# Where the table pieces are halved: one, one, one, three and nine in five bodies instead of three in each

## The chip, the cores and the metric

The kernel runs on one core of a Trainium2 chip. The metric is the device time of one execution in microseconds (us), lower is better; several runs give a median. Engines: PE is TensorE, DVE is VectorE, ACT is ScalarE, POOL is GpSimd, SP is SyncE, which only issues DMAs here.

## The reference

An attention with a recurrent state per head, then two channel stages on its output. B=4, H=8, S=768, D=40:

```
state = 0                                   # per batch and head, D x D
for t in range(S):
    y[t]  = r[t] @ state
    Sa    = state @ a[t]
    state = state * w[t] - outer(Sa, b[t]) + outer(v[t], k[t])
x = y as (B, S, 320)
h = relu(x @ w_in)                          # 320 -> 1024
x = (h * sigmoid(conv3(h))) @ w_out         # 1024 -> 320
u = x + real(fft(fft(x, axis=1), axis=2))
x = u + relu(norm(u) @ w_ch1) @ w_ch2       # 320 -> 1280 -> 320
```

## The kernel before

**Two parts.** `attention` (line 141) runs for the first half of the time, `channels` (line 832) for the rest. The channel stages multiply each operand as a high and a low part (a rounded value and what is left of it), so their weights and Fourier tables have to be split too. That splitting is done during the attention: the tables lie in DRAM side by side (`in_tables`), cut into 17 pieces (`PIECES`, lines 38 and 39): pieces 0 to 12 of 998 columns, piece 13 of 358, pieces 14 to 16 (the last tiles) of 768, all on 128 partitions.

**A piece** takes three jobs. `fetch` (line 344, SP): load it into `w_in`. `halve` (line 433, POOL): `high` = rounded copy (a CAST, L436), then the piece minus `high` in place (L438). `put` (line 352, SP): store `high` (L356) and, after the subtraction, the low part (L358) into the scratch tensors `high_scratch` and `low_scratch`; the last tiles go to `last_scratch` (L360, L362). The place is the buffer of `w` (`w_in`): `piece(i)` (line 263) gives its first and second n columns. It is free between the scans of one step's `w` and the load of the next `w`. `fetch` waits until all scans so far are done (`s_decay`) and until all earlier puts have landed (`s_put`, 32 per piece); `load_w` (line 284) waits for the puts too.

**The attention in bodies.** Time is cut into 6 steps of 128 tokens, each of two chunks of 64. `attention_jobs` (line 80) makes one list of jobs from four words lists: `START`, then `STEP` once for each of g = 0 to 4 (the five *bodies*), then `LAST`. The list is written out by hand and says for every engine in which order it works: each engine walks through the whole list and does its own share, so a job that waits holds all later jobs of its engine. The first number of a word is the step relative to g: `sat:0` belongs to step g, `ta:1` to the preparation of step g+1, `scan:2` to step g+2. Words for steps past the last are dropped, so the fifth body has no scan, `at`, `keys`, `gram`, `decays` and no loads for them. PSUM has six rotating banks, taken in list order.

What stands near the change, by step and chunk:

- `xn` (xi): TensorE multiplies `z` and `kb_tok` (L806), VectorE adds the state (L571), then POOL multiplies it by `w_end` (L445) and counts `s_x`. Four quarters per chunk.
- `xt` (L826, TensorE, transposes of xi) waits for two of the chunk's four POOL products (line 823), the second for four. `sat` (L784, TensorE) of the next chunk: its first half needs two, its second half four (line 780).
- `sub`: VectorE's elimination, 31 pairs of L544 and L546 per step; `unsplit` its two transposes (L553, L558). `diag`: POOL (L456) and ACT (L621) copy `inv_d` into `inv_t`. `mj` (L752), `mt` (L761) and `pu` (L772) follow on TensorE; `pu` needs both copies. `sat` of the next step follows `pu`.
- `keys` (L432, POOL): `kb` times `after`, and `at` (L422, POOL): `a` times `decay`, both before `gram` (L735, TensorE).
- `st` (L799), `y` (L819, L821; VectorE L578) and, on SP, the stores of y for the second chunk (L380). `chunk`: SP loads `rt` and `zt` of the next chunk (L279, L280), once `y` of this chunk is in PSUM.
- `tables` in `LAST` (line 383): SP loads y back and, after all puts, the first weights from the scratch tensors.

In the fifth body the pieces 14, 15 and 16 stand as fetch:0, fetch:1 and fetch:2 do in every body: on POOL `halve:0` behind the four `xn` of the first chunk, `halve:1` ahead of the last three `xn` of the second, `halve:2` behind `diag`. In the numbering of the jobs:

```
number = n[0] + 2 + 3 * g if g >= 0 else n[0]
if number < len(PIECES):
    out.append((stage, 0, 0, number))
```

Of the kernel before, what the change touches and what calls it, by code (L numbers as in the profile page):

```python
# [8 lines left out]
F32 = mybir.dt.float32  # L9
F32R = mybir.dt.float32r  # L10
FP8 = mybir.dt.float8e4

NB, NH, S, D = 4, 8, 768, 40
# [4 lines left out]
STEPS = S // (2 * C)  # L18
# [19 lines left out]
PIECES = [("whole", lo, min(lo + 998, WHOLE)) for lo in range(0, WHOLE, 998)]  # L38
PIECES += [("last", lo, lo + 768) for lo in range(0, LAST_TILES, 768)]

# [26 lines left out]
sub:2 decays:2:0:2 pu:1:1:3 sub:2 pu:1:1:2 xt:0:1:1 sub:2 pu:1:0:3 sub:2 sub:2 sub:2 sub:2 sub:2 pu:1:0:2 sub:2 sub:2  # L70
sub:2 pu:1:1:1 weights:3:0:0 chunk:1:1:0 sub:2 sub:2 sub:2 sub:2
"""
LAST = """
sat:0:0:0 sat:0:0:1 sa:0:0:1 st:0:0:0 sa:0:0:0 xn:0:0:1 xn:0:0:0 sa:0:0:2 st:0:0:1 y:0:0:0 tables:0:0:0 sat:0:1:0
sa:0:0:3 y:0:0:1 st:0:1:0 xt:0:0:0 xn:0:0:2 xn:0:0:3 y:0:1:0 st:0:0:3 st:0:0:2 y:0:0:3 y:0:0:2 rows:0:0:0 sat:0:1:1
# [4 lines left out]
def attention_jobs():  # L80
    solved = [0] * STEPS

    def jobs(words, g):
        out = []
        for word in words.split():
            stage, *numbers = word.split(":")
            n = [int(x) for x in numbers]
            step = g + n[0]
            if stage in ("fetch", "halve", "put"):
                number = n[0] + 2 + 3 * g if g >= 0 else n[0]  # L90
                if number < len(PIECES):
                    out.append((stage, 0, 0, number))
            elif step >= STEPS:
                continue
            elif stage == "sub":
                out.append((stage, step, 0, solved[step]))
                solved[step] += 1
            else:
                job = (stage, step, n[1], n[2])
                out.append(("part", job, n[3], 2) if len(n) > 3 else job)  # L100
        return out

    order = jobs(START, -1)
    for g in range(STEPS - 1):
        order += jobs(STEP, g)
    order += jobs(LAST, STEPS - 1)


    families = {}
    for job in order:  # L110
        if job[0] in UNITS or job[0] in COUNTED:
            families.setdefault(job[:2] if job[0] == "pu" else job[:3], []).append(job)
    numbered = {}
    for family in families.values():
        numbered.update(zip(family, sorted(family, key=lambda job: (job[3], job[2]))))
    return [("part", numbered[job[1]], *job[2:]) if job[0] == "part" else numbered.get(job, job) for job in order]
# [24 lines left out]
def attention(nc, ctx, dram, tables, kept):  # L141
# [4 lines left out]
    def sem(name):  # L146
        return ctx.enter_context(nc.semaphore(name))
# [58 lines left out]
    s_at = sem("s_at")  # L206
# [13 lines left out]
    s_chain = sem("s_chain")  # L220
    s_x = sem("s_x")

    s_fetch = sem("s_fetch")
    s_phigh = sem("s_phigh")
    s_plow = sem("s_plow")
    s_put = sem("s_put")
    s_xin = [sem(f"s_xin{i}") for i in range(2)]
    s_x0hi = sem("s_x0hi")

# [33 lines left out]
    def piece(i):  # L263
        table, lo, hi = PIECES[i]
        n = hi - lo
        return table, lo, hi, w_in[:, 0:n], w_in[:, n:2 * n].bitcast(F32R)

    block = ctx.enter_context(nc.Block())

# [1 line left out]
    def _(sp):  # L271
# [12 lines left out]
        def load_w(g):  # L284
            if g:

                sp.wait_ge(s_decay, NB * g)
            if g > 1:
                fill_of(sp, ("pu", g - 2, 1, NB - 1))
            if halved[0]:  # L290
                sp.wait_ge(s_put, 32 * halved[0])
            for b in range(NB):
                cols = slice(b * NH * SEG + (b > 0), (b + 1) * NH * SEG + 1)
                sp.dma_start(w_in[:, cols], dram["w"][g, :, cols]).then_inc(s_w[b], 16)
# [42 lines left out]
        for stage, g, c, b in whole:  # L337
# [6 lines left out]
            if stage == "fetch":  # L344

                sp.wait_ge(s_decay, NB * scanned)
                if b:
                    sp.wait_ge(s_put, 32 * b)
                table, lo, hi, x, high = piece(b)
                sp.dma_start(x, dram["tables"][:, lo + (WHOLE if table == "last" else 0):hi + (WHOLE if table == "last" else 0)]  # L350
                             ).then_inc(s_fetch, 16)
            if stage == "put":
                table, lo, hi, x, high = piece(b)
                sp.wait_ge(s_phigh, b + 1)
                if table == "whole":
                    sp.dma_start(dram["high"][:, lo:hi], high.bitcast(F32)).then_inc(s_put, 16)  # L356
                    sp.wait_ge(s_plow, b + 1)
                    sp.dma_start(dram["low"][:, lo:hi], x).then_inc(s_put, 16)  # L358
                else:
                    sp.dma_start(dram["last"][0:64, lo:hi], high[0:64].bitcast(F32)).then_inc(s_put, 16)  # L360
                    sp.wait_ge(s_plow, b + 1)
                    sp.dma_start(dram["last"][64:128, lo:hi], x[64:128]).then_inc(s_put, 16)  # L362
                halved[0] += 1
            if stage == "scan":
                scanned = g + 1
# [17 lines left out]
            if stage == "tables":  # L383

                fill_of(sp, ("pu", STEPS - 1, 1, NB - 1))
                sp.wait_ge(s_at, 2 * STEPS)
                sp.wait_ge(s_bt, NB * STEPS)
                sp.wait_ge(s_wp, NB * STEPS)
                sp.wait_ge(s_end, 2 * STEPS)
                load_rows(0)  # L390
                sp.wait_ge(s_put, 32 * len(PIECES))
                for k, part in enumerate(("high", "low")):
                    sp.dma_start(w1[:, k, 0:2, :].rearrange("p t f -> p (t f)").bitcast(F32), dram[part][:, 0:W1]).then_inc(s_w1, 16)
                sp.dma_start(w1[:, 0, 2, :].bitcast(F32), dram["last"][:, 0:FF]).then_inc(s_w1, 16)
# [8 lines left out]
    def _(pool):  # L403
# [9 lines left out]
        for job in whole:  # L413
# [18 lines left out]
                    nc.gpsimd.tensor_tensor(x, x, by, ALU.mult).then_inc(done, 1)  # L432
            elif stage == "halve":
                table, lo, hi, x, high = piece(b)
                pool.wait_ge(s_fetch, 16 * (b + 1))
                nc.gpsimd.tensor_copy(high, x).then_inc(s_phigh, 1)  # L436
                pool.wait_ge(s_phigh, b + 1)
                nc.gpsimd.tensor_tensor(x.bitcast(F32R), x, high.bitcast(F32), ALU.subtract).then_inc(s_plow, 1)  # L438
            elif stage == "xn":

                drain_of(pool, job)
                pool.wait_ge(s_end, 2 * (g + c) + 2)
                state = xi[0:D, b * NH:(b + 1) * NH, 0:D]
                ends = w_end[:, (g + c) % 2, b * NH:(b + 1) * NH, 1 - c]
                nc.gpsimd.tensor_tensor(state, state, ends.unsqueeze(2).broadcast_to([D, NH, D]),  # L445
                                        ALU.mult).then_inc(s_x, 1)
            elif stage == "diag":

                pool.wait_ge(s_zero, 2)
                pool.wait_ge(s_inv, g + 1)  # L450
                if g:

                    fill_of(pool, ("pu", g - 1, 1, NB - 1))
                for cc in range(2):
                    p = C * cc
                    nc.gpsimd.tensor_copy(inv_t_pairs[p:p + Q, :, :, cc, 0:Q], inv_d_slots(p, cc)).then_inc(s_diag_low, 1)  # L456
                    pool.wait_ge(s_diag_low, 2 * g + cc + 1)
# [1235 lines left out]
```

## Time and profile before

| | us |
|---|---|
| median of 3 runs (932.67 to 942.92) | 937.42 |
| the profiled execution | 942.25 |
| its span, first to last instruction | 940.5 |
| busy: PE, DVE, ACT, POOL | 859.7, 610.7, 412.8, 179.5 |
| attention, up to the start of the channel part | about 464.4 |

A row of a timeline gives the start, the time from the first start to the last end, engine, line, operation, tiles written and read, and how many instructions were merged; in brackets how long the engine idled before and what ended that. PEclk is the granted TensorE clock as a share of 2.4 GHz. A landing time of a DMA counts from its issue. A DMA's own duration on SP is how long the issue held the queue. Body 1 runs from about 94.5 to 165.5 us, body 2 to 234.5, body 3 to 306, body 4 to 376.5 and body 5 to 434.5.

### The profile page before, as it was taken

What the parts mean: (1) busy time and instruction counts of PE and PEld (TensorE: products, weight loads), DVE (VectorE), ACT (ScalarE), POOL (GpSimd) and SP (SyncE); (2) the same over time, 40 slices, a digit from 0 to 9 for tenths busy, and PEclk for the clock granted to TensorE, in tenths of its full rate; (3) what the DMA queues carried; (4) which work ended last, traced back from release to release, by engine and by line L of the source; (5) the groups of instructions that cost most, each with busy time, mean ns of one, the idle gap of its engine ahead of it and who ended that gap; (6) DMA issues with size and microseconds to landing.
All of it is one profiled execution on the core that took longest, in us unless ns stands there. A gap on an engine that the chain in (4) does not pass through costs nothing.

```text
span 940.5 us, 26345 instructions
## 1 busy us (share of the span) xinstructions
PE 859.7 (91%) x11113; PEld 819.8 (87%) x11113; DVE 610.7 (65%) x1215; ACT 412.8 (44%) x784; POOL 179.5 (19%) x195
## 2 busy tenths in 40 slices
PE   0769989989989989989899899999999999999998
PEld 0669878888889889979888799999999999999998
DVE  8895877877877876551476746757367574775522
ACT  1565337337346346334266245632455234652311
POOL 5260381381371380240000000000000000000000
PEclk9878999999997997978999999999999999999999
DMA  9751473574564572254880010000100020000000
GB/s 314 218 184 47 144 248 135 187 249 166 175 233 150 186 236 89 49 160 139 299 342 1 1 52 22 1 1 27 47 22 1 1 72 1 22 2 1 22 22 22
DMA packets 58677, 100.79 MB, mean 107 GB/s; under 512 B 28529, under 2 KB 40562, under 8 KB 54898
## 3 DMA queue, kind: packets, MB, share of 16 engines
q1 hardware_dynamic: 58562, 99.11, 32.0%
q8 instruction: 90, 1.47, 0.7%
q14 instruction: 25, 0.20, 0.1%
HBM read 76.40 MB, written 22.70 MB: 105 GB/s over the span
## 4 chain that ended last, share of the span: by engine, by line
PE 40%; DVE 8%; ACT 1%; issue 1%; DVEq 0%; ACTq 0%
PE psum L1393 19%; PE psum L1453 9%; PE psum L1419 8%; PE psum L1473 2%; DVE stats L1262 1%; PE psum L1489 1%; DVE res L1272 1%; DVE hid L1208 1%; DVE res L1253 1%; DVE tok L1264 1%; DVE xn L1197 1%; DVE cv L1285 1%; DVE res L1254 1%; DVE cv L1283 1%; DVE gs L1203 0%
## 5 line engine op out<-in xcount | busy, mean ns | idle before, releaser
L1393 PE MATMUL psum<-xn,w 128*128 128x384 f32 x640 | 125.1, 339 | 0.2 <-DVE xn L1197 0.2
L1393 PEld LDWEIGHTS psum<-xn,w 128*128 128x128 f32 x640 | 110.5, 188 | 1.1 <-issue 0.6
L1393 PE MATMUL psum<-xs,w 128*128 128x384 f32 x512 | 97.3, 343 | 5.9 <-PEq L1604 3.7
L1393 PEld LDWEIGHTS psum<-xs,w 128*128 128x128 f32 x512 | 91.5, 194 | 6.3 <-issue 6.3
L1419 PE MATMUL psum<-w,gs 128*128 128x320 f32 x576 | 90.0, 310 | 4.2 <-DVE gs L1203 4.1
L1419 PEld LDWEIGHTS psum<-w,gs 128*128 128x128 f32 x576 | 86.3, 188 | 5.9 <-DVE gs L1203 5.9
L735 PE MATMUL bank<-at,kb 64*64 64x64 f32 x1536 | 51.8, 238 | 36.7 <-DVE kb L506 21.3
L735 PEld LDWEIGHTS bank<-at,kb 64*64 64x64 f32 x1536 | 47.0, 148 | 40.4 <-issue 33.3
L445 POOL TENSOR_TENSOR xi<-xi,w_end 40x320 f32<-40x320 f32 x44 | 31.0, 723 | 208.1 <-DVE xi L571 177.1
L546 DVE TENSOR_TENSOR inv<-inv,outer 128x31 f32<-128x31 f32 (+15 forms) x186 | 64.9, 349 | 6.4
L563 DVE TENSOR_TENSOR score<-bank,mask 128x512 f32<-128x512 f32 x48 | 32.7, 690 | 55.2 <-PE bank L799 54.5
L1283 DVE SCALAR_TENSOR_TENSOR cv<-hp,conv,cv 128x768 f32<-128x768 f32 x32 | 32.6, 1018 | 52.4 <-ACT cv L1094 52.4
L544 DVE TENSOR_TENSOR outer<-low,inv 128x31 f32<-128x31 f32 (+15 forms) x186 | 62.4, 335 | 5.0
L772 PE MATMUL bank<-inv_t,rhs 128*80 128x128 f32 x384 | 60.0, 327 | 3.1 <-issue 3.1
L1453 PE MATMUL psum<-w,hid 128*128 128x320 f32 x360 | 59.9, 311 | 2.3 <-DVE res L1272 1.3
L1453 PE MATMUL psum<-w,gs 128*128 128x320 f32 x360 | 60.0, 311 | 0.0
L772 PEld LDWEIGHTS bank<-inv_t,rhs 128*80 128x80 f32 x384 | 55.9, 188 | 4.4 <-issue 3.8
L1453 PEld LDWEIGHTS psum<-w,hid 128*128 128x128 f32 x360 | 54.9, 188 | 4.6 <-DVE hid L1208 2.8
L432 POOL TENSOR_TENSOR kb<-kb,after 128x512 f32<-128x512 f32 x44 | 53.5, 1243 | 20.0 <-DMA kb<-in_kb 19.9
L1453 PEld LDWEIGHTS psum<-w,gs 128*128 128x128 f32 x360 | 55.4, 188 | 1.2 <-DVE gs L1208 1.0
L1208 DVE SCALAR_TENSOR_TENSOR gs<-psum,gs 128x384 fp32r<-128x384 f32 x40 | 22.3, 557 | 52.0 <-ACT gs L1073 52.0
L799 PE MATMUL bank<-rt,zt 128*128 128x128 f32 x384 | 53.7, 284 | 0.5 <-DVE y_t L578 0.5
(129 smaller groups left out, 1674.9 us busy)
## 6 DMA issues: line engine op xcount, KB each, us to landing
kb<-in_kb SPq DMA_DIRECT2D x24, 512.0 KB, 8.2
rt<-in_rt SPq DMA_DIRECT2D x12, 1024.0 KB, 8.5
w_in<-in_tables SPq DMA_DIRECT2D x13, 499.0 KB, 3.6
high_scratch<-w_in SPq DMA_DIRECT2D x13, 499.0 KB, 3.3
low_scratch<-w_in SPq DMA_DIRECT2D x13, 499.0 KB, 3.8
at<-in_a SPq DMA_DIRECT2D x6, 1024.0 KB, 4.9
zt<-in_vt SPq DMA_DIRECT2D x12, 512.0 KB, 9.6
w_in<-in_w SPq DMA_DIRECT2D x18, 260.0 KB, 4.5
```

The source lines that it names most:

```text
L432: nc.gpsimd.tensor_tensor(x, x, by, ALU.mult).then_inc(done, 1)
L544: link(nc.vector.tensor_tensor(prod, low[:, b + 1:Q, b:b + 1].broadcast_to([128, n, m]), inv[:, b:b + 1, 0:m].broadcast_to([128, n, m]), A ...
L546: link(nc.vector.tensor_tensor(inv[:, b + 1:Q, 0:m], inv[:, b + 1:Q, 0:m], prod, ALU.add))
L563: nc.vector.tensor_tensor(score[:, b * NH:(b + 1) * NH, :], bank, mask[:, :].unsqueeze(1).broadcast_to([128, NH, C]), ALU.mult).then_inc(d ...
L735: last = mm(out[C * cc:C * cc + C, i, :], kb[r, n, cc, c, :], at_chunks[r, n, cc, :], start=True, stop=True)
L772: last = mm(t[0:2 * D, 128 * i:128 * i + 128], rhs[:, h, :], inv_t[:, h, :, :], start=True, stop=True)
L799: last = mm(t[:, 128 * i:128 * i + 128], zt[:, c, n, :], rt[:, c, n, :, :], start=True, stop=True)
L1208: nc.vector.scalar_tensor_tensor(hid[q % 2][:, f % 2, 1, :], ps[6 + f % 2][:, 0:HALF], 0.0, f32(hid[q % 2][:, f % 2, 0, :]), ALU.max, ALU. ...
L1283: link(nc.vector.scalar_tensor_tensor(cv[:, :], h[:, 1:S + 1], conv[:, f, 1:2], cv[:, :], ALU.mult, ALU.add))
L1393: last = mm(ps[bank][:, 0:HALF], a[:, 128 * f:128 * f + 128], y[:, HALF * half:HALF * (half + 1)], start=(i == 0), stop=(i == len(every) - 1))
L1419: last = mm(ps[t][:, 0:DM], gs[:, f % 2, x, 128 * t:128 * t + 128], w2[:, y, f, :], start=(f == 0 and m == 0), stop=(f == NF - 1 and m == 2))
L1453: last = mm(ps[HALVES[k]][:, 0:DM], hid[h][:, f % 2, x, 128 * k:128 * k + 128], w4[:, y, f, :], start=(f == 0 and m == 0), stop=(f == NC - ...
```

## The change

The pieces keep their order and their jobs. The start still does two. Bodies 1, 2 and 3 do one each, at the place of their old fetch:0, halve:0 and put:0. Body 4 does three, in the old places. Body 5 does nine (pieces 8 to 16) and has its own list, `LATE`, in which the other jobs stand in the same order as in `STEP`. Since no `w` and no `decay` is needed any more then, the nine take turns in two places, `w_in` and `decay`, with a semaphore each for fetch and put. A fetch waits for the earlier puts of its own place only; one into `decay` also waits for all `decays` copies (`s_wp`) and all `at` products (`s_at`).

```diff
--- before.py
+++ after.py
@@ -37,6 +37,10 @@
 WHOLE, LAST_TILES = W1 + W2 + DFT_S + DFT_D + W3 + W4, FF + FC
 PIECES = [("whole", lo, min(lo + 998, WHOLE)) for lo in range(0, WHOLE, 998)]
 PIECES += [("last", lo, lo + 768) for lo in range(0, LAST_TILES, 768)]
+
+BY_STEP = (2, 1, 1, 1, 3, 9)
+TURNS = sum(BY_STEP[:-1])
+assert len(PIECES) == sum(BY_STEP)
 
 
 
@@ -70,6 +74,19 @@
 sub:2 decays:2:0:2 pu:1:1:3 sub:2 pu:1:1:2 xt:0:1:1 sub:2 pu:1:0:3 sub:2 sub:2 sub:2 sub:2 sub:2 pu:1:0:2 sub:2 sub:2
 sub:2 pu:1:1:1 weights:3:0:0 chunk:1:1:0 sub:2 sub:2 sub:2 sub:2
 """
+LATE = """
+fetch:0 fetch:1 sat:0:0:0 ta:1:0:0 halve:0 put:0 sat:0:0:1 sa:0:0:1 ta:1:0:1 tb:1:1:3 sa:0:0:0 ta:1:0:3 ta:1:0:2
+st:0:0:0:0 st:0:0:0 fetch:2 halve:1 put:1 akv:1:0:0:0 akv:1:0:0 st:0:0:1:0 st:0:0:1 sa:0:0:3 tb:1:1:2 akv:1:0:1:0
+akv:1:0:1 st:0:0:2:0 xn:0:0:0 fetch:3 halve:2 put:2 st:0:0:2 st:0:0:3:0 akv:1:0:2:0 akv:1:0:2 st:0:0:3 akv:1:0:3:0
+sub:1 sa:0:0:2 tb:1:1:1 tb:1:1:0 fetch:4 halve:3 put:3 akv:1:0:3 xn:0:0:2 xn:0:0:1 xn:0:0:3 y:0:0:0:0 y:0:0:0
+y:0:0:1:0 y:0:0:1 sub:1 tb:1:0:0 fetch:5 halve:4 put:4 tb:1:0:1 y:0:0:2:0 y:0:0:2 xt:0:0:1 tb:1:0:3 sub:1 sat:0:1:1
+sub:1 sub:1 sub:1 fetch:6 halve:5 put:5 sub:1 sat:0:1:0 sub:1 y:0:0:3:0 y:0:0:3 chunk:1:0:0 xt:0:0:0 sa:0:1:0 sa:0:1:1
+fetch:7 halve:6 put:6 sa:0:1:3 st:0:1:1:0 xn:0:1:0 st:0:1:1 sub:1 tb:1:0:2 sa:0:1:2 st:0:1:0:0 st:0:1:3:0 sub:1
+fetch:8 halve:7 put:7 st:0:1:0 st:0:1:2:0 st:0:1:2 st:0:1:3 sub:1 xn:0:1:1 sub:1 xn:0:1:2 xn:0:1:3 y:0:1:0:0 halve:8
+put:8 y:0:1:1:0 y:0:1:2:0 y:0:1:1 y:0:1:0 sub:1 sub:1 sub:1 unsplit:1:0:0 y:0:1:2 y:0:1:3:0 y:0:1:3 diag:1:0:0
+mj:1:0:0:0 mj:1:0:1:0 mj:1:0:1 mj:1:0:0 mt:1:0:0:0 mt:1:0:0 xt:0:1:0 pu:1:0:0 pu:1:1:0 mt:1:0:1:0 mt:1:0:1 pu:1:0:1
+pu:1:1:3 pu:1:1:2 xt:0:1:1 pu:1:0:3 pu:1:0:2 pu:1:1:1 chunk:1:1:0
+"""
 LAST = """
 sat:0:0:0 sat:0:0:1 sa:0:0:1 st:0:0:0 sa:0:0:0 xn:0:0:1 xn:0:0:0 sa:0:0:2 st:0:0:1 y:0:0:0 tables:0:0:0 sat:0:1:0
 sa:0:0:3 y:0:0:1 st:0:1:0 xt:0:0:0 xn:0:0:2 xn:0:0:3 y:0:1:0 st:0:0:3 st:0:0:2 y:0:0:3 y:0:0:2 rows:0:0:0 sat:0:1:1
@@ -87,9 +104,8 @@
             n = [int(x) for x in numbers]
             step = g + n[0]
             if stage in ("fetch", "halve", "put"):
-                number = n[0] + 2 + 3 * g if g >= 0 else n[0]
-                if number < len(PIECES):
-                    out.append((stage, 0, 0, number))
+                if n[0] < BY_STEP[g + 1]:
+                    out.append((stage, 0, 0, sum(BY_STEP[:g + 1]) + n[0]))
             elif step >= STEPS:
                 continue
             elif stage == "sub":
@@ -101,8 +117,9 @@
         return out
 
     order = jobs(START, -1)
-    for g in range(STEPS - 1):
+    for g in range(STEPS - 2):
         order += jobs(STEP, g)
+    order += jobs(LATE, STEPS - 2)
     order += jobs(LAST, STEPS - 1)
 
 
@@ -220,10 +237,10 @@
     s_chain = sem("s_chain")
     s_x = sem("s_x")
 
-    s_fetch = sem("s_fetch")
+    s_fetch = [sem(f"s_fetch{i}") for i in range(2)]
     s_phigh = sem("s_phigh")
     s_plow = sem("s_plow")
-    s_put = sem("s_put")
+    s_put = [sem(f"s_put{i}") for i in range(2)]
     s_xin = [sem(f"s_xin{i}") for i in range(2)]
     s_x0hi = sem("s_x0hi")
 
@@ -263,7 +280,15 @@
     def piece(i):
         table, lo, hi = PIECES[i]
         n = hi - lo
-        return table, lo, hi, w_in[:, 0:n], w_in[:, n:2 * n].bitcast(F32R)
+        where = decay if turn(i) else w_in
+        return table, lo, hi, where[:, 0:n], where[:, n:2 * n].bitcast(F32R)
+
+    def turn(i):
+        return (i - TURNS) % 2 if i >= TURNS else 0
+
+    def fellows(i):
+
+        return sum(turn(k) == turn(i) for k in range(i + 1))
 
     block = ctx.enter_context(nc.Block())
 
@@ -288,7 +313,7 @@
             if g > 1:
                 fill_of(sp, ("pu", g - 2, 1, NB - 1))
             if halved[0]:
-                sp.wait_ge(s_put, 32 * halved[0])
+                sp.wait_ge(s_put[0], 32 * halved[0])
             for b in range(NB):
                 cols = slice(b * NH * SEG + (b > 0), (b + 1) * NH * SEG + 1)
                 sp.dma_start(w_in[:, cols], dram["w"][g, :, cols]).then_inc(s_w[b], 16)
@@ -344,22 +369,25 @@
             if stage == "fetch":
 
                 sp.wait_ge(s_decay, NB * scanned)
-                if b:
-                    sp.wait_ge(s_put, 32 * b)
+                if turn(b):
+                    sp.wait_ge(s_wp, NB * STEPS)
+                    sp.wait_ge(s_at, 2 * STEPS)
+                if fellows(b) > 1:
+                    sp.wait_ge(s_put[turn(b)], 32 * (fellows(b) - 1))
                 table, lo, hi, x, high = piece(b)
                 sp.dma_start(x, dram["tables"][:, lo + (WHOLE if table == "last" else 0):hi + (WHOLE if table == "last" else 0)]
-                             ).then_inc(s_fetch, 16)
+                             ).then_inc(s_fetch[turn(b)], 16)
             if stage == "put":
                 table, lo, hi, x, high = piece(b)
                 sp.wait_ge(s_phigh, b + 1)
                 if table == "whole":
-                    sp.dma_start(dram["high"][:, lo:hi], high.bitcast(F32)).then_inc(s_put, 16)
+                    sp.dma_start(dram["high"][:, lo:hi], high.bitcast(F32)).then_inc(s_put[turn(b)], 16)
                     sp.wait_ge(s_plow, b + 1)
-                    sp.dma_start(dram["low"][:, lo:hi], x).then_inc(s_put, 16)
+                    sp.dma_start(dram["low"][:, lo:hi], x).then_inc(s_put[turn(b)], 16)
                 else:
-                    sp.dma_start(dram["last"][0:64, lo:hi], high[0:64].bitcast(F32)).then_inc(s_put, 16)
+                    sp.dma_start(dram["last"][0:64, lo:hi], high[0:64].bitcast(F32)).then_inc(s_put[turn(b)], 16)
                     sp.wait_ge(s_plow, b + 1)
-                    sp.dma_start(dram["last"][64:128, lo:hi], x[64:128]).then_inc(s_put, 16)
+                    sp.dma_start(dram["last"][64:128, lo:hi], x[64:128]).then_inc(s_put[turn(b)], 16)
                 halved[0] += 1
             if stage == "scan":
                 scanned = g + 1
@@ -388,7 +416,8 @@
                 sp.wait_ge(s_wp, NB * STEPS)
                 sp.wait_ge(s_end, 2 * STEPS)
                 load_rows(0)
-                sp.wait_ge(s_put, 32 * len(PIECES))
+                for k in range(2):
+                    sp.wait_ge(s_put[k], 32 * sum(turn(i) == k for i in range(len(PIECES))))
                 for k, part in enumerate(("high", "low")):
                     sp.dma_start(w1[:, k, 0:2, :].rearrange("p t f -> p (t f)").bitcast(F32), dram[part][:, 0:W1]).then_inc(s_w1, 16)
                 sp.dma_start(w1[:, 0, 2, :].bitcast(F32), dram["last"][:, 0:FF]).then_inc(s_w1, 16)
@@ -432,7 +461,7 @@
                     nc.gpsimd.tensor_tensor(x, x, by, ALU.mult).then_inc(done, 1)
             elif stage == "halve":
                 table, lo, hi, x, high = piece(b)
-                pool.wait_ge(s_fetch, 16 * (b + 1))
+                pool.wait_ge(s_fetch[turn(b)], 16 * fellows(b))
                 nc.gpsimd.tensor_copy(high, x).then_inc(s_phigh, 1)
                 pool.wait_ge(s_phigh, b + 1)
                 nc.gpsimd.tensor_tensor(x.bitcast(F32R), x, high.bitcast(F32), ALU.subtract).then_inc(s_plow, 1)
```

## Rows read from the trace of the kernel before

**Rows 1.** Busy time by stretch; columns: stretch, length, busy of each engine (instructions), PEclk, DMA share, GB/s.
```profile
94.50:165.50 71.00, 63.80 (x1394) 58.95 (x1390) 55.12 (x114) 33.69 (x69) 29.88 (x26) 0.98 0.53 179
165.50:234.50 69.00, 64.39 (x1411) 59.33 (x1407) 54.92 (x114) 33.57 (x69) 29.87 (x26) 0.98 0.60 197
234.50:306.00 71.50, 67.45 (x1390) 62.49 (x1388) 54.66 (x113) 33.93 (x69) 29.90 (x26) 0.90 0.57 188
...
376.50:434.50 58.00, 53.42 (x1036) 50.29 (x1035) 25.55 (x56) 20.91 (x41) 15.52 (x16) 0.85 0.33 84
```

**Rows 2.** Timeline of POOL, second body: the first halving, the last keys.
```profile
183.42 1.02 POOL L436 CAST w_in<-w_in 128x998 fp32r<-128x998 f32 x1 [0.73 <-DMA w_in<-in_tables]
184.51 1.96 POOL L438 TENSOR_TENSOR w_in<-w_in 128x998 fp32r<-128x998 f32 x1
...
200.29 2.34 POOL L432 TENSOR_TENSOR kb<-kb,after 128x512 f32<-128x512 f32 x2 [2.01 <-DMA kb<-in_kb]
```

**Rows 3.** Timeline of SP, second body: the last `kb` load and the next fetch.
```profile
191.39 5.33 SPq L312 DMA_DIRECT2D kb<-in_kb  x1
196.82 1.35 SPq L350 DMA_DIRECT2D w_in<-in_tables  x1
```

**Rows 4.** Timeline of POOL, fifth body: the xi products and the diagonal copy.
```profile
383.05 0.72 POOL L445 TENSOR_TENSOR xi<-xi,w_end 40x320 f32<-40x320 f32 x1 [28.49 <-DVE xi L571]
389.29 2.10 POOL L445 TENSOR_TENSOR xi<-xi,w_end 40x320 f32<-40x320 f32 x3 [5.51 <-DVE xi L571]
...
415.24 2.12 POOL L456 COPY inv_t<-inv_d 32x1024 f32<-32x1024 f32 x2 [4.06 <-issue]
```

**Rows 5.** Timeline of PE, fifth body: xt, sat, mj and the first pu.
```profile
393.61 0.69 PE L826 MATMUL bank<-ident,xi 40*128 40x40 f32 x8
...
394.82 2.08 PE L784 MATMUL bank<-pu,xi 80*64 80x64 f32 x64
...
413.52 3.47 PE L752 MATMUL bank<-inner,gram_m 32*32 32x32 f32 x128 [2.63 <-DVE inner L553]
...
421.86 3.67 PE L772 MATMUL bank<-inv_t,rhs 128*80 128x128 f32 x16 [0.30 <-issue]
```

**Rows 6.** Timeline of SP, fifth body: two fetches, rt ahead of the second, rt after the last pu.
```profile
371.76 3.65 SPq L350 DMA_DIRECT2D w_in<-in_tables  x1
...
397.84 0.34 SPq L279 DMA_DIRECT2D rt<-in_rt  x1
...
398.91 3.81 SPq L350 DMA_DIRECT2D w_in<-in_tables  x1
...
435.35 0.36 SPq L279 DMA_DIRECT2D rt<-in_rt  x1
```

**Rows 7.** Single DMAs and their landing times, issued near 144, 286, 372 and 399.
```profile
low_scratch<-w_in SPq DMA_DIRECT2D x1, 499.0 KB, 5.2
...
low_scratch<-w_in SPq DMA_DIRECT2D x1, 499.0 KB, 2.6
...
w_in<-in_tables SPq DMA_DIRECT2D x1, 384.0 KB, 7.1
...
w_in<-in_tables SPq DMA_DIRECT2D x1, 384.0 KB, 7.4
```

**Rows 8.** The page's DMA issues: median time to landing over 13 pieces.
```profile
w_in<-in_tables SPq DMA_DIRECT2D x13, 499.0 KB, 3.6
...
low_scratch<-w_in SPq DMA_DIRECT2D x13, 499.0 KB, 3.8
```

**Rows 9.** Timeline of DVE: one shape of sub, in the second and the fifth body.
```profile
184.92 0.40 DVE L544 TENSOR_TENSOR outer<-low,inv 128x231 f32<-128x231 f32 x1
...
395.91 0.40 DVE L544 TENSOR_TENSOR outer<-low,inv 128x231 f32<-128x231 f32 x1
```

**Rows 10.** Two stretches of PE alone: stretch, length, busy, PEclk, DMA share, GB/s.
```profile
281.00:295.00 14.00, 13.46 (x200) 0.52 0.38 134
...
414.00:431.00 17.00, 15.05 (x282) 0.50 0.24 65
```

## The prediction

> **What bounds the kernel now.** I read the busy time by stretch first, one stretch per body. TensorE is busy for 63.8 of 71.0 us in the first body, 64.4 of 69.0 in the second and 67.45 of 71.5 in the third: it idles 7.2, 4.6 and 4.0 us. In the fifth it is busy 53.4 of 58.0 us, beside 25.6 us of VectorE and only 15.5 us of GpSimd [rows 1]. So TensorE's own list of jobs sets the time, and another engine counts only where its result comes after TensorE wants it. That is why the rest is read in order of time: for each job on GpSimd and on the queue of SyncE, when it ends and when TensorE asks for it. The profiled execution took 942.25 us (span 940.5, 1.75 around it), the median is 937.42; a shift read in the span is added to the median. A measurement of this kernel can tell about 1% (9.4 us) from no change.
>
> **The first three bodies: two pieces fewer in each.** What stays is the piece at fetch:0, whose halving stands ahead of GpSimd's work on `at` and `kb`. What goes is halve:1 and halve:2. One halving is a cast of 1.02 and a subtraction of 1.96 us, 3.0 together [rows 2], so six of them are 18 us of GpSimd, with three times 0.5 MB of DMA each. Is any of it waited for? The one thing of that part of a body that TensorE needs is the last quarter of `kb`, for which GpSimd waits 2.01 us in the second body [rows 2]. But that load is issued at 191.39 and holds the queue for 5.33 us, and the second piece's fetch goes out behind it, at 196.82 [rows 3]; the pieces that go are all behind the wait, and the one in front of it stays. The halvings that go stand in front of three xi products and the low diagonal copy, or behind it; in the fifth body, with its halvings in the same places, that copy still has 4.5 us of slack [rows 4, 5]. I take 0 for the three bodies. Bounds: a loss has no mechanism there, so 0 at the most above; the gain is bounded by TensorE's 15.8 us of idle time in them [rows 1], far from 0, and this belongs to a rival below. The fourth body keeps three pieces in the old places: 0.
>
> **The fifth body: nine instead of three.** The list without fetch, halve and put is word for word the old one, so only the nine pieces and what waits behind them on SyncE and GpSimd change. Two xi events of the old run matter, because both stand on GpSimd behind halvings now.
>
> First event. GpSimd did the first xi product at 383.05 and the other three from 389.29, 2.10 us in all [rows 4]. TensorE's first xt of this body (two products needed) began at 393.61, the second half of sat (all four) at about 395.9 [rows 5]. Slack: 3.6 and 4.5 us. Now halve:0 and halve:1 stand ahead of the first product, halve:2 and halve:3 ahead of the three. Step by step, with the number of the piece in the list:
> - fetch 0 is issued at 371.76, as now, and holds the queue until 375.4 behind rt and zt [rows 6]. It landed after 7.1 us with 384 KB [rows 7]; with 499 KB I take 7.5: 379.3. Halve 0 ends at 382.3. Fetch 1 (the second place, `decay`) needs nothing but decays and `at` of the last step, both long done; halve 1 ends at 385.3, the first product at 386.0. Nobody waits for that one.
> - put 0 (low half) goes at 382.3 and takes 3.8 [rows 8]: 386.1. Only then may fetch 2 go, 3.6 us [rows 8]: 389.7. Halve 2 ends 392.7.
> - put 1 is issued by SyncE only behind fetch 2. Its low half leaves about 0.8 after that fetch, behind 1 MB of the queue. Bounds: 2.6 alone, 7.1 behind rt and zt; I take 5.2, a low half measured with traffic near it [rows 7]. So put 1 lands 6.0 after fetch 2's issue: 392.1. Fetch 3: 395.7. Halve 3 ends 398.7.
> - The second product of the body ends at 399.4, the fourth at 400.8. TensorE's xt starts 399.4 instead of 393.6: **5.8 us of waiting**. Sat's second half would then stand at 401.7, and is covered.
> VectorE doesn't take this back: after the shift it waits for TensorE's results in the old order, and TensorE still waits 2.63 us for its transpose before mj [rows 5].
>
> Second event. The low diagonal copy ran 415.24 to 417.4 on GpSimd [rows 4], pu wanted it at 421.86 [rows 5]: slack 4.5. Going on with 6.0 per fetch and put, and a second place in between:
> - put 2 398.1, fetch 4 401.7, halve 4 404.7; put 3 404.1, fetch 5 (358 columns, estimated 2.9) 407.0, halve 5 (in proportion 1.3) 408.3; put 4 410.1, fetch 6 (768 columns) 413.7, halve 6 (2.7, estimated between proportion and whole) 416.4.
> - rt and zt for the last step now leave SyncE behind put 5, about 411.4, instead of 397.84; they are wanted in the last body and have time. Fetch 7 stands behind them. Before, the fetch issued 1.07 after rt held the queue 3.81 us [rows 6] and landed after 7.4 [rows 7], 8.5 after rt. So fetch 7 lands 419.9, halve 7 ends 422.6, three xi products 424.7.
> - put 6 leaves when that issue is through, 418.6, and lands 422.4; fetch 8 426.0; halve 8 428.7; diagonal copy (2.12) 430.8.
> TensorE, 5.8 late, would start pu at 427.7; it starts at 430.8: **another 3.1 us**. Together the last body starts 8.9 us late. The y stores wait on SyncE behind put 8 and go from about 429 on; the rows and tables they feed are loaded only once the last pu is filled (435.35 before [rows 6], some 444 now), so they stay covered, and so does the wait for all puts.
>
> Ends of the unknown terms: with every put at the 2.6 to 3.8 of the quiet rows [rows 7, 8] the same walk gives 3.2 for the first wait and 0.8 for the second, 4.0 in all. With 7.1 instead of 5.2 for each of the four crowded puts it gives 8.9 + 4 x 1.9 = 16.5. **Sum: 937.4 + 0 + 5.8 + 3.1 = 946.3 us.**
>
> A rule to weigh. While GpSimd ran the subtraction of a halving (184.51 to 186.47) [rows 2], VectorE's product of 128x231 took 0.40 us; the same shape at 395.91, with GpSimd idle, took 0.40 [rows 9]. The Trainium skill (SBUF — State Buffer, "Who interferes with whom") says that a VectorE instruction with both inputs in SBUF and a GpSimd instruction that reads SBUF shut each other out for a whole instruction. This trace doesn't agree: no stretching at all, so the sum has no such term.
>
> **The rivals.**
> - The puts are quick: only the xi wait is left, 4.0 us, 941.4. For it: 2.6 us landings exist. Against: here put and fetch queue behind one another every time.
> - TensorE's clock. Idle of a few us is followed by half speed here: 281 to 295 at 0.52, 414 to 431 at 0.50 [rows 10]. A wait of 5.8 at 393.6 may bring a stretch like the first, 14 us at 0.52, 6.7 us of work lost, before pu. Then pu starts at 421.9 + 5.8 + 6.7 = 434.4, the second wait is covered, +12.5: 949.9. Against: in the forecast up to 3.1 us of that is hidden behind the GpSimd chain, and VectorE limits part of this stretch anyway.
> - The other side, faster: the fetch behind the last `kb` quarter does share the engines with it. Without it `kb` lands earlier by up to the 2.01 us of GpSimd's wait in each of three bodies [rows 2], 6.0; and where TensorE then idles less, the third body's low-clock stretch [rows 10] goes, 6.7 more. 12.7 against 8.9 is -3.8: 933.6. It decides only if both come. Against it: the order of the queue [rows 3].
> - The pieces move and all stays covered: 937.4. This needs halve 3 to end before 393, three landings faster than any row here.
> - GpSimd and VectorE shut each other out. VectorE limits TensorE only in front of the transpose, where halve 4 and 5 run, 4.3 us: 8.9 + 4.3, 950.6. Rows 9 speak against it.
>
> **How the numbers follow.** Forecast 0.45, quick puts 0.17, clock 0.18, faster bodies 0.10, all covered 0.07, shut out 0.03. The forecast lies 0.95% above before, so about half of it counts as slower by over 1% (0.22); with the clock and the shut-out that is 0.40. Faster by over 1% needs the kb rival and a little more: 0.05. Within 1%: 0.55. The forecast's own range is 941.4 to 953.9; the stated one goes down to 936, which leaves out most of the faster case, and up to 954.
>
> **What would show it.** In the changed profile, the first xt of the fifth body comes 3 to 6 us later against sat of that body, with TensorE idle in front, released by GpSimd's xi product; GpSimd waits for the fetches of pieces 2 and 3 in between. The low diagonal copy ends after TensorE has finished mt, and pu waits for it. Bodies one to three stay at 71, 69 and 71.5 us within 1.5 us each, apart from the clock. I am wrong if the xi products come before TensorE wants them, or if those three bodies shrink by more than 2 us each with GpSimd's wait for `kb` gone.

## The result and the profile after

The changed kernel took 945.64 us (median of 12 executions, 936.9 to 953.32), before 936.11 us (12 executions beside it). The ratio is 1.0072, 95% interval 1.0045 to 1.0098. Some executions of a kernel are slow ones (two of the twelve here), and a ratio leaves them out; by the two medians alone it would be 1.010. Measured a second time beside other kernels it gave 1.0089 (1.0054 to 1.0124). So the changed kernel is slower by 0.7 to 0.9%, 7 to 8 us; the medians differ by 9.5 and 10.3 us.

The profiled execution after took 945.71 us with a span of 943.9; the one before had 940.5. The first view to look at is the busy time by stretch, with the stretches cut as in [rows 1], 6 to 7 us behind the `sat` that opens each body (start and end, length, busy of PE, PEld, DVE, ACT, POOL, then PEclk, DMA share, GB/s):

```profile
94.50:162.50 68.00, 63.83 (x1396) 58.81 (x1394) 55.17 (x114) 33.51 (x69) 24.05 (x22) 0.97 0.43 142
162.50:230.50 68.00, 63.64 (x1402) 58.95 (x1400) 54.78 (x114) 33.62 (x69) 24.00 (x22) 0.97 0.48 156
230.50:298.70 68.20, 63.78 (x1396) 58.83 (x1392) 54.60 (x114) 33.61 (x69) 24.00 (x22) 0.97 0.48 150
298.70:369.40 70.70, 65.41 (x1374) 60.62 (x1371) 51.50 (x110) 33.90 (x69) 29.88 (x26) 0.93 0.57 185
369.40:438.00 68.60, 56.41 (x1037) 52.77 (x1036) 25.59 (x56) 20.93 (x41) 31.37 (x28) 0.80 0.61 190
```

Against [rows 1], GpSimd has 6 us less in each of the first three bodies and 16 more in the fifth. From sat to sat the bodies take 68.1, 67.9, 68.3, 71.8 and 75.2 us, before 71.1, 68.6, 71.8, 71.7 and 64.7. The first three are 7.2 us shorter together, the fifth 10.5 longer; behind it both kernels need the same 505.3 us. Of the 7.2 us, 2.9 are idle time of TensorE (15.9 before, 12.9 after) and 4.3 are busy time, at 0.95 of the clock before and 0.97 after. Two executions of one kernel differ by as much as that gain, as shown further down, so the profile alone proves only the loss.

The timeline of GpSimd in the fifth body shows the chain:

```profile
378.06 0.72 POOL L474 TENSOR_TENSOR xi<-xi,w_end 40x320 f32<-40x320 f32 x1
382.09 1.01 POOL L465 CAST w_in<-w_in 128x998 fp32r<-128x998 f32 x1 [3.31 <-DMA w_in<-in_tables]
383.19 1.95 POOL L467 TENSOR_TENSOR w_in<-w_in 128x998 fp32r<-128x998 f32 x1
390.10 1.01 POOL L465 CAST decay<-decay 128x998 fp32r<-128x998 f32 x1 [4.96 <-DMA decay<-in_tables]
391.19 1.95 POOL L467 TENSOR_TENSOR decay<-decay 128x998 fp32r<-128x998 f32 x1
393.10 2.09 POOL L474 TENSOR_TENSOR xi<-xi,w_end 40x320 f32<-40x320 f32 x3
...
416.86 0.82 POOL L465 CAST decay<-decay 128x768 fp32r<-128x768 f32 x1 [5.46 <-DMA decay<-in_tables]
417.77 1.81 POOL L467 TENSOR_TENSOR decay<-decay 128x768 fp32r<-128x768 f32 x1
419.54 2.09 POOL L474 TENSOR_TENSOR xi<-xi,w_end 40x320 f32<-40x320 f32 x3
421.58 0.81 POOL L465 CAST w_in<-w_in 128x768 fp32r<-128x768 f32 x1
422.47 1.81 POOL L467 TENSOR_TENSOR w_in<-w_in 128x768 fp32r<-128x768 f32 x1
424.22 2.12 POOL L485 COPY inv_t<-inv_d 32x1024 f32<-32x1024 f32 x2
```

GpSimd stands idle for 4.96 us ahead of the fourth halving, waiting for its DMA, and the three xi products stand behind it. In [rows 4] they ran as soon as VectorE had added the state. TensorE pays for it (timeline of PE, the rows with a wait; xt, mj, mt, pu):

```profile
393.96 1.05 PE L855 MATMUL bank<-ident,xi 40*128 40x40 f32 x8 [6.93 <-POOL xi L474]
...
419.70 3.06 PE L781 MATMUL bank<-inner,gram_m 32*32 32x32 f32 x128 [2.64 <-DVE inner L582]
424.84 1.92 PE L790 MATMUL bank<-inv_d,inner 32*32 32x32 f32 x64 [2.08 <-ACT inner L697]
...
428.06 3.28 PE L801 MATMUL bank<-inv_t,rhs 128*80 128x128 f32 x16 [0.30 <-issue]
```

The wait ahead of xt is 6.93 us (none in [rows 5]). The wait ahead of pu isn't there: the diagonal copy ends at 426.34, TensorE arrives at 428.06. It arrives late because its clock fell during the first wait and stayed low behind it (stretch, length, busy, PEclk, DMA share, GB/s):

```profile
383.00:394.00 11.00, 3.82 (x94) 0.81 0.56 174
394.00:408.00 14.00, 14.00 (x156) 0.54 0.71 238
```

The clock is at half speed until 406.9. The kernel before has full speed from 366.0 to 413.8 and half speed from there to 430.9 (see [rows 10]); after, that second stretch is shorter, 420.6 to 430.8. So pu starts 13.3 us later within its body than before, and 2.8 us of that are won back behind it. Of the 10.5 us by which the fifth body grew, 6.9 are the wait, 2.9 more busy time of TensorE (63.0 us against 60.1), and 0.7 other waits.

### The profile page after: what moved, and what is told of

Same layout as the page of the kernel before. It is cut to its first block, busy times and chain, and to the rows that moved or that the text cites. A ratio compares the mean times of both kernels' runs of the same rounds, so it can differ in the third digit from the quotient of the medians.

```text
span 943.9 us, 26345 instructions
## 1 busy us (share of the span) xinstructions
PE 857.0 (91%) x11113; PEld 816.8 (87%) x11113; DVE 610.8 (65%) x1215; ACT 412.0 (44%) x784; POOL 179.7 (19%) x195
## 4 chain that ended last, share of the span: by engine, by line
PE 40%; DVE 8%; ACT 1%; issue 1%; DVEq 0%; ACTq 0%
PE psum L1422 19%; PE psum L1482 9%; PE psum L1448 8%; PE psum L1502 2%; DVE stats L1291 1%; PE psum L1518 1%; DVE res L1301 1%; DVE hid L1237 1%; DVE res L1282 1%; DVE tok L1293 1%; DVE xn L1226 1%; DVE cv L1314 1%; DVE res L1283 1%; DVE cv L1312 1%; DVE gs L1232 0%
## 5 line engine op out<-in xcount | busy, mean ns | idle before, releaser
L575 DVE TENSOR_TENSOR inv<-inv,outer 128x31 f32<-128x31 f32 (+15 forms) x186 | 64.9, 349 | 6.4
L801 PE MATMUL bank<-inv_t,rhs 128*80 128x128 f32 x384 | 56.3, 314 | 3.7 <-issue 3.7
L801 PEld LDWEIGHTS bank<-inv_t,rhs 128*80 128x80 f32 x384 | 52.5, 179 | 4.9 <-issue 4.3
```

The lines of the kernel that those rows point to most:

```text
L575: link(nc.vector.tensor_tensor(inv[:, b + 1:Q, 0:m], inv[:, b + 1:Q, 0:m], prod, ALU.add))
L801: last = mm(t[0:2 * D, 128 * i:128 * i + 128], rhs[:, h, :], inv_t[:, h, :, :], start=True, stop=True)
```

## The experiments

All ratios are to the kernel before, run on the same chip in turns.

**1. The loss alone.** Three pieces stay in bodies 1 to 3, and the fifth does the nine of the changed kernel.

```diff
-BY_STEP = (2, 1, 1, 1, 3, 9)
+PIECES = PIECES[0:14] + PIECES[8:17]
+BY_STEP = (2, 3, 3, 3, 3, 9)
```

> Bodies 1 to 4 keep three pieces each as before; the fifth does the nine of the changed kernel (pieces 8 to 16, of which 8 to 13 are done a second time with the same values). Bodies are measured from sat to sat on TensorE: before 71.1, 68.6, 71.8, 71.7, 64.7 us, after 68.1, 67.9, 68.3, 71.8, 75.2. Theory (the gain in bodies 1 to 3 comes from the pieces that are gone): bodies 1 to 3 as before, sum 209 to 214, the fifth 74 to 77, so 9 to 12 us slower than before, and some 7 slower than the changed kernel minus noise of 3. Rival (the shorter bodies are luck of TensorE's clock in one execution): no difference from the changed kernel beyond noise, 5 to 8 us slower than before.

Measured: 1.0139 (1.0099 to 1.0180), six executions. Bodies 72.4, 72.2, 68.8, 68.1, 72.0. The first three sum to 213.4, as expected. The fifth is shorter than the 74 to 77 expected, while the total, 13 us, is just over the 9 to 12 expected.

> loss_only again. First measurement 1.0139 (1.0099 to 1.0180) on six runs. Theory by the steps of the prediction: 8.9 us or 1.0095; what the profiles show beyond it, a crowded put of 7.5 us instead of 5.2 and half speed behind the first wait, allows up to 1.015. In the profile a wait of 5.5 to 7.5 us ahead of the first xt.

Measured: 1.0093 (1.0056 to 1.0129). Bodies 70.2, 68.0, 68.4, 68.4, 74.1. Both are slower than before by 9 to 13 us, and both profiles have both waits, ahead of xt and of pu: 5.91 and 0.99 us in the first, 6.82 and 1.88 in the second:

```profile
391.12 1.04 PE L856 MATMUL bank<-ident,xi 40*128 40x40 f32 x8 [6.82 <-POOL xi L475]
...
423.86 3.67 PE L802 MATMUL bank<-inv_t,rhs 128*80 128x128 f32 x16 [1.88 <-POOL inv_t L486]
```

**2. The gain alone.** One piece in bodies 1 to 3, three in the fourth and fifth, six not done. The diff leaves out the stores of constants that fill the place of the six, and that the fifth body has the old list again.

```diff
-BY_STEP = (2, 1, 1, 1, 3, 9)
+PIECES = [PIECES[i] for i in (0, 1, 2, 5, 8, 11, 12, 13, 14, 15, 16)]
+BY_STEP = (2, 1, 1, 1, 3, 3)
```

> One piece in each of bodies 1 to 3, three in the fourth and fifth as before; the six pieces that have gone are not done at all, their columns of the scratch tensors are filled with constants in the start (12 stores of 0.5 MB), so the output is not the reference's. Theory: bodies 1 to 3 take 68 us each, sum 203 to 206 against 211.5 before, the fifth 64 to 66, total 5 to 8 us faster than before. Rival (clock luck): sum 208 to 214, total within 2 us of before.

Measured: 0.9981 (0.9951 to 1.0011). Bodies 67.1, 71.3, 71.3, 71.2, 62.0. The first three sum to 209.7 and the total is 2 us from before: this measurement alone is what the rival expected.

> gain_only again. First measurement 0.9981 (0.9951 to 1.0011). Theory (less traffic in bodies 1 to 3, fewer stops of TensorE in the middle of a job): 0.994 to 0.999; rival (no gain at all): 0.999 to 1.002.

Measured: 0.9950 (0.9915 to 0.9984). Bodies 70.9, 68.0, 68.3, 71.8, 64.8. The mean of both is 0.9966, 3 us. There is a gain, smaller than the 7.2 us of the one profile, and below the 5 to 8 us first expected.

**3. Which part of a piece costs time in bodies 1 to 3.** Both kernels are built so that the part that stays is at its old place.

```diff
 halves_stay: as gain_only
+                if stage == "halve" and 0 <= g < 3 and n[0] > 0:
+                    out.append(("idle", 0, 0, 2 * g + n[0] - 1))
 ...
+            elif stage == "idle":
+                nc.gpsimd.tensor_copy(high, x).then_inc(s_ihigh, 1)
 ...
+                nc.gpsimd.tensor_tensor(x.bitcast(F32R), x, high.bitcast(F32), ALU.subtract).then_inc(s_ilow, 1)
 traffic_stays: (2, 3, 3, 3, 3, 3), BARE = (3, 4, 6, 7, 9, 10)
 ...
             elif stage == "halve":
+                if b in BARE:
+                    continue
```

> As gain_only, but GpSimd does the six halvings in bodies 1 to 3 at their old places, on what lies in w_in, with no fetch and no put (same computation left out as there). Theory A (the gain comes from the DMA traffic of the pieces, which delays TensorE's instruction fetch and other loads): as gain_only, sum of bodies 1 to 3 203 to 206. Theory B (the gain comes from GpSimd's time, behind which xi products and the diagonal copy stand): as before, 209 to 213, total 0 to 2 us from before.

Measured: 0.9958 (0.9930 to 0.9987). Bodies 67.7, 68.0, 68.2, sum 203.9, as theory A expected.

> Three pieces in every body as before, but for the second and third piece of bodies 1 to 3 GpSimd does nothing: they are fetched and put without being halved, so the low part is the whole value and the high part is stale and the output is not the reference's. Theory A (traffic): as before, sum of bodies 1 to 3 209 to 213, total within 2 us of before. Theory B (GpSimd's time): sum 203 to 206, total 5 to 8 us faster.

Measured: 1.0032 (0.9998 to 1.0066). Bodies 74.9, 75.0, 70.6, sum 220.4. That is well over the 209 to 213 expected: the granted clock of this one execution was 0.89, 0.89 and 0.95 in them, so the sum says little and the time decides. The time is 3 us over before, where at most 2 were expected; its interval reaches down to no change.

The two ratios were measured on one chip and their intervals don't meet. Theory A: the 18 us of GpSimd's work cost nothing, the DMA traffic does. Where, the list of waits of TensorE says (us in total, times, longest). Over 94 to 305 us, before:

```profile
PE bank L735 <- issue: 4.9, 4, 1.9
PE bank L752 <- issue: 2.3, 3, 1.1
```

traffic_stays, the same two jobs (gram and mj):

```profile
PE bank L773 <- issue: 8.9, 6, 2.8
PE bank L790 <- issue: 3.5, 3, 1.8
```

halves_stay (gram is L787, mj L804):

```profile
PE bank L787 <- issue: 1.5, 3, 1.0
...
PE bank L804 <- issue: 1.2, 2, 1.0
```

These are stops in which TensorE waits for no semaphore that the profile shows, and they stand in the middle of a job. Before, first body:

```profile
129.68 0.56 PE L735 MATMUL bank<-at,kb 64*64 64x64 f32 x10
132.02 0.44 PE L735 MATMUL bank<-at,kb 64*64 64x64 f32 x6 [1.78 <-issue]
...
139.55 1.26 PE L752 MATMUL bank<-inner,gram_m 32*32 32x32 f32 x67
141.50 1.14 PE L752 MATMUL bank<-inner,gram_m 32*32 32x32 f32 x61 [0.70 <-issue]
```

After, same place:

```profile
129.76 0.56 PE L764 MATMUL bank<-at,kb 64*64 64x64 f32 x10
131.28 0.44 PE L764 MATMUL bank<-at,kb 64*64 64x64 f32 x6 [0.96 <-issue]
...
137.33 1.26 PE L781 MATMUL bank<-inner,gram_m 32*32 32x32 f32 x67
139.46 1.14 PE L781 MATMUL bank<-inner,gram_m 32*32 32x32 f32 x61 [0.87 <-issue]
```

The job is cut at the same instruction in both kernels (10 and 6, 67 and 61), whatever the length of the stop. All stops without a releaser in bodies 1 to 3 add up to 11.7, 13.9, 8.9 and 14.1 us in the four profiles with three pieces (before, loss_only twice, traffic_stays), and to 4.6 to 6.0 us in the nine with one (5.4 and 6.0 in the changed kernel, 5.9, 5.5 and 5.3 in gain_only twice and halves_stay). In each sum 1.3 to 2.1 us stand ahead of the first pu of a body, whatever the traffic.

What ends the others can be read from the traces. The page of the kernel before lists, beside the queue that moves the data, a DMA queue of another kind, with packets of 16 KB:

```profile
q1 hardware_dynamic: 58562, 99.11, 32.0%
q8 instruction: 90, 1.47, 0.7%
```

In bodies 1 to 3 such a packet comes about every 6 us. Over all thirteen profiles the timeline of TensorE from 86 to 450 us shows 141 stops without a releaser other than those ahead of pu, of 0.15 to 2.83 us, and every one of them ends 1.19 to 1.65 us after the end of a packet of this queue. The stop of 1.78 us above ends at 132.02, its packet ran from 129.78 to 130.71. The stop of 0.96 us ends at 131.28, its packet ran from 128.97 to 129.90. The packet took 0.93 us both times, it only began 0.8 us later. So TensorE stands there for want of its next instructions. Why the packet begins later where the traffic is heavier, no run here shows.

Not all of this is paid. From three pieces to one the stops shrink by 6.7 us in the mean of the profiles, but all idle time of TensorE in bodies 1 to 3 only from 15.6 to 13.3 us (means of four and nine profiles): where TensorE stops less, it waits longer for others, in the changed profile 2.3 us instead of 0.8 for ScalarE's copy of `gram_m`. That is the size of the 3 us in the times.

**4. Is it one wait or a chain?** The fourth halving alone moved behind the three xi products.

```diff
-... tb:1:1:0 fetch:4 halve:3 put:3 akv:1:0:3 xn:0:0:2 xn:0:0:1 xn:0:0:3 ...
+... tb:1:1:0 fetch:4 put:3 akv:1:0:3 xn:0:0:2 xn:0:0:1 xn:0:0:3 halve:3 ...
```

> The changed kernel, with only the halving of the fifth body's fourth piece (halve:3) moved from ahead of that body's last three xi products of the first chunk to behind them. Theory (two gates on one self-timed chain of fetch, halve and put): the wait of 6.9 us ahead of xt goes, but the low diagonal copy stays behind halve:8, which ends near 424 whatever TensorE does, so pu waits instead; the fifth body 72 to 75 us against 75.2 after, 0 to 3 us faster than the changed kernel. Rival (only the first wait mattered, the slack of 4.5 us of the diagonal copy holds): fifth body 65 to 67 us, 8 to 10 us faster than the changed kernel.

Measured: 1.0075 (1.0046 to 1.0103), the changed kernel's time. Its profile is of an execution with a span of 953.7, far above its median, so only who waits for whom is read from it:

```profile
396.86 0.66 PE L855 MATMUL bank<-ident,xi 40*128 40x40 f32 x8 [0.49 <-POOL xi L474]
...
429.53 1.05 PE L855 MATMUL bank<-ident,xi 40*128 40x40 f32 x8 [4.96 <-POOL xi L474]
435.72 3.67 PE L801 MATMUL bank<-inv_t,rhs 128*80 128x128 f32 x16 [5.15 <-POOL inv_t L485]
```

The first wait is 0.49 us instead of 6.93, no low clock follows it (1.00 from 390 to 410 us), and its time comes back at the next two places where TensorE meets a product that stands behind a halving. The chain of fetch, halve and put runs at its own pace; removing one gate moves the wait to the next.

**5. All gates.** halve:2 and halve:3 behind the xi products, halve:6, 7 and 8 behind the diagonal copy; fetches and puts untouched. The cut shows where they stand now; each is still done once.

```diff
-... xn:0:0:3 ...
+... xn:0:0:3 halve:2 halve:3 ...
-... diag:1:0:0 ...
+... diag:1:0:0 halve:6 halve:7 halve:8 ...
```

> The changed kernel, with halve:2 and halve:3 behind the xi products of the first chunk and halve:6, halve:7 and halve:8 behind the low diagonal copy in GpSimd's order; fetches and puts keep their order on SyncE. Theory: no halving that waits for a DMA stands ahead of a product that TensorE wants; the fifth body takes 64 to 67 us, both waits gone, all puts landed by about 425, ahead of the load of the tables; 8 to 11 us faster than the changed kernel, and 1 to 4 us faster than before. Rival (the traffic of six more pieces itself stops TensorE in the fifth body, as it did in bodies 1 to 3): fifth body 68 to 72 us.

Measured: 0.9989 (0.9960 to 1.0018). Bodies 67.9, 71.5, 68.2, 75.2, 63.6.

> all_moved again, beside late_place on the same chip. Fifth body 63 to 66 us with no wait on GpSimd's products; total within 3 us of before.

Measured: 1.0010 (0.9976 to 1.0045). Bodies 68.1, 67.7, 68.2, 68.3, 64.3. The fifth body is as short as before with the nine pieces in it, GpSimd's products are no longer waited for, and the rival (68 to 72 us) is out. The kernel is 6 to 9 us faster than the changed one by the ratios, and not to be told from the one before.

The gain of 1 to 4 us over before, as expected, did not come, although gain_only and halves_stay (0.9981, 0.9950, 0.9958) have it with the same one piece in bodies 1 to 3. Part of the cost went along with the pieces: the stops without a releaser in the fifth body are 1.0 and 1.7 us here against 0.3 before, and behind that body the kernel needs 506.1 us in both profiles, against 505.3. The rest is no larger than the intervals and stays open.

These two profiles are of one and the same kernel, and its fourth body took 75.2 in one and 68.3 in the other. The stretch of that body (length, busy of PE, PEclk, DMA share, GB/s), first all_moved, then all_moved_b:

```profile
294.40:369.60 75.20, 69.44 (x1395) 0.89 0.54 179
```

```profile
291.00:359.40 68.40, 63.98 (x1394) 0.98 0.61 197
```

The clock was granted for 0.89 and for 0.98 of full speed: 69.4 us of busy time against 64.0, for the same matmuls. A body of this kernel that takes 71 or 75 us instead of 68 is no evidence on a change.

**6. The one piece at a quieter place.**

```diff
-                if n[0] < BY_STEP[g + 1]:
+                if 0 <= g < 3:
+                    if n[0] == 2:
+                        out.append((stage, 0, 0, sum(BY_STEP[:g + 1])))
+                elif n[0] < BY_STEP[g + 1]:
```

> As all_moved, and the one piece of bodies 1, 2 and 3 is done at the old place of the third (fetch:2, halve:2 behind the diagonal copy, put:2) instead of the first. Theory (what TensorE loses in these bodies is the DMA traffic of pieces in the stretch of kb loads and short matmuls): GpSimd's waits for kb shrink from 2.0, 1.5 and 2.3 us to under 1 each, bodies 1 to 3 take 66 to 68 us each, total 2 to 5 us faster than all_moved, so 3 to 6 faster than before. Rival: one piece at that place stops TensorE in mj and mt instead, sum of bodies 1 to 3 within 2 us of all_moved, no difference in time.

Measured: 0.9988 (0.9958 to 1.0017), medians 936.61 and 937.63 for all_moved_b beside it. Bodies 70.3, 66.3, 71.3. GpSimd's waits for `kb` are 1.69, 0.92 and 1.92 us, against 2.45, 2.49 and 3.65 in all_moved_b: shorter, and nothing in the time follows from it. TensorE's stops without a releaser in bodies 1 to 3 are 4.7 us, against 4.6 and 5.5 in the two profiles of all_moved, so the new place doesn't spare them. The expected 2 to 5 us were a miss.

**7. Do the parts add up?**

> The changed kernel again, beside loss_only and gain_only on one chip, to see whether the two parts add up. If they do: its ratio to before is that of loss_only plus that of gain_only minus 1, within 0.004. First measurement 1.0072, so 1.004 to 1.010.

Measured: 1.0089 (1.0054 to 1.0124). Means of two measurements each: loss 1.0116, gain 0.9966, sum less one 1.0082; changed kernel 1.0081. Over all measurements they add up: about 11 us lost in the fifth body, 3 won in the first three. The last three, taken on one chip, do so less well: 1.0093 and 0.9950 would give 1.0043, which is 0.0046 from 1.0089 and so just outside the 0.004 expected. Each ratio is known to about 0.0035, so this doesn't contradict the sum, but it doesn't show it either, and it leaves the 3 us uncertain by as much.

## Why the prediction was right, and where not

The forecast was 946.3, measured 945.64; in change, 8.9 us against 6.7 and 8.3 by the two ratios, 9.5 and 10.3 by the medians. Its main mechanism, GpSimd's products held up behind halvings that wait for their DMAs, is the one seen. Point by point:

- **The first event, 5.8 us.** The wait is there, on the product named, and measures 6.93, 5.91, 6.82 and 5.54 us in four profiles with the nine pieces (after, loss_only twice, changed_b). The walk through the chain can be laid beside the changed profile, in which fetch 0 is issued 7.2 us earlier (364.55):

| start of | predicted, less 7.2 | measured |
|---|---|---|
| halve 0 | 372.1 | 372.06 |
| halve 2 | 382.5 | 382.09 |
| halve 3 | 388.5 | 390.10 |
| halve 4 | 394.5 | 396.77 |
| halve 6 | 406.5 | 408.01 |
| halve 7 | 412.7 | 416.86 |
| end of the diagonal copy | 423.6 | 426.34 |

- **The put behind a fetch, taken at 5.2 us, was sized too small.** The DMAs issued at 378.66 and at 387.12:

```profile
low_scratch<-decay SPq DMA_DIRECT2D x1, 499.0 KB, 7.4
...
low_scratch<-w_in SPq DMA_DIRECT2D x1, 499.0 KB, 5.5
```

Alone, a low half landed in 2.6 us here too (issued at 375.14). The first crowded one is at the upper end that [rows 7] gave for a DMA behind rt and zt, the next two took 5.5 and 5.8 us and the fourth, behind the short fetch, 4.1.
- **One link of the chain was left out.** The walk sends fetch 7 out 1.07 us behind rt. It goes into `decay` and has to wait for put 5, which lands there: rt is issued at 405.78, put 5 lands at 409.7, fetch 7 is issued at 409.76. That is 3 us more than the walk has, and it accounts for halve 7 being 4.2 us late where halve 6 was 1.5.
- **The second event, 3.1 us, was named rightly but is not paid in the changed kernel.** The wait of pu is 0 in after and changed_b, 0.99 in loss_only, 1.88 in loss_only_b. What differs is the clock: in all four it fell to half speed while TensorE stood ahead of xt, and it stayed there for another 13, 12, 8 and 7 us. The longer it stayed, the later TensorE came to pu by itself. With one_moved's wait of 0.49 us, and in the kernel before with none, that stretch ran at 1.00. So forecast and clock rival are one event: the wait brings the low clock, and a long low clock hides the second wait. In the changed profile pu starts 13.3 us later in its body, near the clock rival's 12.5 and not the forecast's 8.9; that the body grew by less is due to the shorter second stretch at half speed, which neither of them had. That the second gate exists is seen in one_moved, where pu waits 5.15 us.
- **The size of the loss.** The fifth body grew by 10.5 (after), 11.2 (changed_b), 7.3 and 9.4 us (loss_only twice) over the 64.7 of the one profile of before, mean 9.6, and the times of loss_only give 11: the 8.9 was one to two short. Four more profiles with the old fifth body have 62.0, 64.8, 64.9 and 64.6 us.
- **0 for bodies 1 to 3 failed, by some 3 us.** The step that failed is the question "is any of it waited for?", asked only of GpSimd's work and of the last `kb` load. Both answers hold: halves_stay shows the work to be free, and the wait for `kb` stayed (2.19, 2.01 and 3.73 us before; 1.96, 1.46 and 2.29 in the changed profile; 2.73, 3.20 and 1.96 in changed_b). What I left out is that the traffic itself makes TensorE stop in the middle of jobs, for packets of instructions that come later. The rows were in reach: the stops of 1.78 and 1.88 us in the first body carried no releaser, and I counted them as idle time without asking what ended it.
- **The two errors cancel.** 3 us too little gain, about 2 too little loss; that the sum lies so near the time is partly luck. So is the last digit: the sum starts from 937.4, and before measured 936.11 beside the changed kernel.
- **A slip in the chances.** 0.22 for the forecast with 0.18 for the clock and 0.03 for the shut-out is 0.43, not 0.40.
- **GpSimd against VectorE.** The price of 0 holds: VectorE is busy for 25.6 us in the fifth body before and after, with twice the GpSimd work beside it.
- **The faster side.** Its mechanism was not seen: GpSimd's wait for `kb` is 2.2 us shorter in the sum of three bodies in the changed profile, but the same as before in changed_b (7.9 us), and TensorE's time doesn't follow it in late_place either. A gain for another reason was seen.

## What to carry to other kernels

Work that waits for a DMA must not stand on an in-order engine ahead of work that a busier engine wants; and where several such places hang on one self-paced chain, all have to be moved, since moving one hands its wait to the next. Work that is "hidden" by its engine's idle time still has to be priced by its traffic. One profile can't tell a few us in a stretch where the clock comes and goes: time the parts apart, twice.

## What the runs showed of the hardware that I had not expected

- TensorE stops at fixed instructions, mostly in the middle of a job of short matmuls, for 0.15 to 2.8 us. All 141 such stops in thirteen profiles end 1.19 to 1.65 us after a 16 KB packet of a DMA queue of kind "instruction". With those ahead of pu they come to 8.9 to 14.1 us in three bodies with three pieces each, and to 4.6 to 6.0 with one.
- A 0.5 MB store took 2.6 us to land alone and 7.4 behind a fetch and another store on the same queue.
- The granted clock fell to half speed in each of the four waits of 5.5 to 6.9 us ahead of xt, and stayed there for 7 to 13 us of work behind them.
- The same body of the same kernel took 68.3 and 75.2 us in two executions, at 0.98 and 0.89 of the clock.
